# Taking the filler matmuls and the state's identity matmul off TensorE, and adding the state on VectorE instead

## What is computed

```
for t in range(S):                     # B,H,S,D = 4,8,768,48
    new_re = ar * S_re - ai * S_im     # a normalised to |a| <= 0.999, S_* are D x D
    new_im = ar * S_im + ai * S_re
    S_re, S_im = (new_re + outer(k[t], v[t]), new_im)
    y[t] = q[t] @ S_re
x = y as rows (3072 x 384)
x = dense_mixture(x)                   # all 8 experts, normalised gates
out = routed_mixture(x)                # one expert for each row
```

## Time and profile before

| | |
|---|---|
| device time, median of 3 runs | 2652.64 us |
| lowest, highest | 2652.48, 2661.65 us |
| the profiled execution | 2661.65 us, span 2659.8 us |
| mean granted TensorE clock | 0.957 |
| TensorE matmul busy over the span | 2469.9 us (93%) |
| VectorE, ScalarE, GpSimd busy | 1152.1, 748.4, 188.2 us |

### The profile page before, as it was taken

The page is one execution under the profiler, slowest core; times in us unless marked ns, Lnnn a source line. Parts: engine busy times, 40 slices in busy tenths (PEclk is TensorE's granted clock), DMA queues, the critical chain, the costliest instruction groups (busy, mean ns, idle before and its releaser), DMA issues. The chain is left out here.

```text
span 2659.8 us, 41528 instructions
## 1 busy us (share of the span) xinstructions
PE 2469.9 (93%) x14282; PEld 2301.4 (87%) x14283; DVE 1152.1 (43%) x2517; ACT 748.4 (28%) x1293; POOL 188.2 (7%) x176
## 2 busy tenths in 40 slices
PE   0499899999999999999999999999999999599998
PEld 0266666678999999999999999999999999488897
DVE  6876667533444333333333333333333332475433
ACT  4555555332111211211211211211221212254322
POOL 0000000000110110110110110110110100022221
PEclk9988887897999999999999999999999999699999
DMA  3102111110000000000000000000000011243210
GB/s 120 36 29 71 43 66 48 33 34 25 24 25 0 24 25 0 24 24 0 24 24 0 24 24 0 24 24 0 24 24 0 24 37 41 101 144 131 78 38 21
DMA packets 44717, 96.81 MB, mean 36 GB/s; under 512 B 4101, under 2 KB 26651, under 8 KB 44640
## 3 DMA queue, kind: packets, MB, share of 16 engines
q1 hardware_dynamic: 40672, 84.97, 9.4%
q0 software_dynamic: 3968, 10.82, 1.3%
HBM read 161.83 MB, written 10.81 MB: 65 GB/s over the span
## 5 line engine op out<-in xcount | busy, mean ns | idle before, releaser
L986 PE MATMUL bank<-x_parts,w_hi 128*128 (+1 forms) x3072 | 783.4, 335 | 0.1
L871 ACT ACTIVATE h_hi<-bank 128x384 fp32r<-128x384 f32 x512 | 250.2, 492 | 1250.2 <-PE bank L986 1250.1
L986 PEld LDWEIGHTS bank<-x_parts,w_hi 128*128 128x128 f32 x3072 | 554.2, 188 | 0.2 <-DVEq L908 0.2
L940 DVE SCALAR_TENSOR_TENSOR h_lo<-bank,h_hi 128x384 fp32r<-128x384 f32 x512 | 284.1, 557 | 574.5 <-ACT h_hi L871 574.5
L986 PE MATMUL bank<-x_parts,w_lo 128*128 (+1 forms) x1536 | 513.8, 335 | 0.0
L998 PE MATMUL bank<-w_hi,h_hi 128*128 128x384 f32 x1536 | 513.3, 334 | 0.0
L998 PE MATMUL bank<-w_hi,h_lo 128*128 128x384 f32 x1536 | 513.1, 334 | 0.0
L998 PE MATMUL bank<-w_lo,h_hi 128*128 128x384 f32 x1536 | 513.0, 334 | 0.0
L960 DVE SCALAR_TENSOR_TENSOR mixed<-bank,gate,mixed 128x384 f32 (+1 forms) x336 | 207.7, 618 | 444.9 <-PE bank L998 444.9
L986 PEld LDWEIGHTS bank<-x_parts,w_lo 128*128 128x128 f32 x1536 | 289.0, 188 | 0.0
L998 PEld LDWEIGHTS bank<-w_lo,h_hi 128*128 128x128 f32 x1536 | 288.3, 188 | 0.0
(11 more groups left out here) (198 smaller groups left out, 2238.2 us busy)
## 6 DMA issues: line engine op xcount, KB each, us to landing
routed_w_raw<-in_moe_w SPq DMA_DIRECT2D x64, 1536.0 KB, 6.5
w_raw<-in_moe_w SPq DMA_DIRECT2D x32, 768.0 KB, 6.1
q_k<-in_qk SPq DMA_DIRECT2D x24, 512.0 KB, 3.6
decay<-in_a SPq DMA_DIRECT2D x20, 528.0 KB, 5.1
v_rows<-in_v SPq DMA_DIRECT2D x24, 192.0 KB, 2.4
mixed_rows<-mixed SPq DMA_DIRECT2D x4, 1152.0 KB, 4.6
decay<-in_a SPq DMA_DIRECT2D x4, 432.0 KB, 4.8
routed_x<-mixed_rows,gather_now POOLq DMA_INDIRECT x31, 3.1
```

The source lines that it names most:

```text
L871: nc.scalar.activation(h_parts[par][0][:, c, :], h_bank[c], ACT.Relu).then_inc(h_hi, 1)
L940: nc.vector.scalar_tensor_tensor(out=h_parts[par][1][:, c, :], in0=h_bank[c], scalar=0.0, in1=h_parts[par][0][:, c, :].bitcast(F32), op0=A ...
L986: last = nc.tensor.matmul(h_bank[c].rearrange("p (u s) -> p u s", u=SUB), w1_parts[half][w][:, k, c * PT:(c + 1) * PT], mem.x[:, bass.ds(b ...
```

## The change

The identity matmul on the old state goes, and every product of k and v is written to its place in the bank on its own (`start=True, stop=True`). VectorE adds the old state to the bank and writes the sum to a new SBUF tile `state_sum`; the two decay products read that tile (for c = 0 they still read the bank). All filler matmuls go: one for each unit that passes a state on (20) and four for each unit but the last (92).

```diff
+    ssum = mem.at("state_sum", [PT, 2, PAIRS, D], F32, mem.after)
...
-            def await_state_sum(u):
+            def add_state(u):
                 if passes_on(u):
                     dve.wait_ge(kv_done, kept(u) + 1)
+                    if u % NCH:
+                        dve.wait_ge(state_ready, kept(u))
+                        nc.vector.tensor_tensor(ssum[:, :, :, :], state[:, u % 2, :, :, :], kv, ALU.add).then_inc(
+                            state_read, 1)
 
             def decay_state(u, t):
                 if passes_on(u):
                     b, c = divmod(u, NCH)
+                    source = kv
+                    if c:
+                        source = ssum[:, :, :, :]
+                        dve.wait_ge(state_read, kept(u) + 1)
...
-                    nc.vector.tensor_tensor(dst[:, :, :, :], kv, across, ALU.mult).then_inc(state_steps, 1)
-                    if t == IM:
+                    nc.vector.tensor_tensor(dst[:, :, :, :], source, across, ALU.mult).then_inc(state_steps, 1)
+                    if t == IM and not c:
                         dve.wait_ge(state_steps, 2 * kept(u) + 2)
                         dve.sem_inc(state_read, 1)
...
-                await_state_sum(u)
+                add_state(u)
...
-            def keep_warm(bank):
-                nc.tensor.matmul(bank[:, :], ident[:, :], ident[:, :].unsqueeze(1).to_broadcast([PT, BANK // PT, PT]),
-                                 start=True, stop=True)
...
-                                            start=c == 0, stop=c == 0 or (part == IM and h >= H - 2))
+                                            start=True, stop=True)
...
-                    if c:
-                        pe.wait_ge(state_ready, kept(u))
-                        nc.tensor.matmul(kvb[:, 0:2 * PAIRS * D], ident[:, :],
-                                         state[:, u % 2, :, :, :].rearrange("p t g e -> p (t g e)"), start=True, stop=False)
...
-                if passes_on(u):
-                    keep_warm(kt_re)
...
-                if u + 1 < UNITS:
-                    for n in range(4):
-                        keep_warm(sc_a)
```

## The result

The changed kernel takes 2676.65 us (median of 7 executions, 2670.18 to 2681.52) against 2656.33 us before (7 executions, 2652.11 to 2663.74): ratio 1.0072, 95% interval 1.0057 to 1.0086. It is slower by 0.72%, some 19 us. The forecast was 44 us, and a time of 2697.

A forecast was written before the change was run, and what follows sets the result against it. Scan units were taken as bound by the ring through VectorE, ScalarE's squares and odd scores, late units by TensorE. All low +73 us, less 29 for recoveries, gave +44 on 2652.6: about 2697, range 2660 to 2728.

The forecast's parts named there:

- rival A: The forecast itself, chance 0.57: clock low most of the time with short recoveries, 2682 to 2712 us, middle 2697.
- low-clock sums: Unit lengths in units 1 to 23 at the low clock: 15.2 us to the sum of squares plus 11.6 to the mask.
- recovery: Rise of the clock at the sum of squares, 3.2 us at full clock, claimed to save 2.6 us.
- +73: Units 1 to 23 all at the low clock: +39 us in units 1 to 16 and +34 in 17 to 23.
- the ring: Path setting a scan unit's length: odd mask, VectorE, ScalarE's squares, sum of squares, odd scores; addition costs 9 us there.
- one in two: Share of the 22 units with a sum of squares taken to have a recovery, giving back 29 us.
- four in nine: Share of sums of squares begun low or behind a pause that came out at full clock before; worth 25 us.
- Scan and late units: Units 1 to 16, where fillers mostly fill a wait, and 17 to 23, where they stand on the path; all low +39, +34.
- B: Rival, chance 0.15: no recoveries to speak of in the first stage, 68 to 73 us slower, about 2724.
- C: Rival, chance 0.08: clock at full as often as before, its mean above about 0.82; faster, about 2638 us.
- D: Rival, chance 0.14: only scan units fall to low clock, late ones without pauses hold full; +14 us, about 2666.

The follow-up runs named there:

- three_adds: Changed kernel with VectorE's addition of the state done three times in each of 16 units, same output; 2699.62 us, ratio 1.0162 to the kernel before.
- five_adds: Changed kernel with VectorE's addition of the state done five times in each of 16 units, same output; 2714.93 us, ratio 1.0207 to the kernel before.
- split_squares: Changed kernel with the sum of squares split: real part, logits, imaginary part, same work; 2717.42 us, ratio 1.0233 to the kernel before.
- squares_fillers: Kernel before with two more fillers (four in a last chunk) ahead of the sum of squares in units 1 to 17; 2633.08 us, ratio 0.9904.
- hold: Kernel before with squares_fillers' extra fillers plus one ahead of the odd scores in units without an identity matmul; 2620.65 us, ratio 0.9860.

## Why the prediction was wrong in size

**Direction and mechanism.** Slower, by the clock, was right. The mean clock of units 1 to 23 is 0.59 and 0.58, where rival A had near 0.6. Behind the odd scores it is low in 22 of the 23 units from 1 on (all but unit 1; in unit 17 it falls 0.8 us behind the odd mask).

**The low-clock sums.** They are right in the part from the sum of squares to the odd mask: 11.6 us, and the missed units of three_adds and five_adds have 11.64. The part ahead of it was 0.5 us too long, 15.2 where 14.73 was measured; a unit without a recovery comes to 26.4, not 26.8. Unit 11 of the changed kernel, at 0.50, has 25.23 where I had 25.7. Unit 23 has 18.83 us at 0.50 where I had 21.4: that sum seems to have kept the 1.9 us of k transposes, which a last chunk doesn't have. With the lengths as measured (a recovered unit with 2.6 us added), all units low would be +66.7 us and not +73.

**The parts on the ring.** The instruction was sized rightly, 0.55 against 0.54, and the decay products have no change; but I put the 0.55 us on the ring whole (9 us in all), and it costs 0.04. The wait for the release of the bank, which the edit takes away for c > 0, had a part in no sum. The statement that operand sources in SBUF and in the bank take the same 0.55 us had no row of that length behind it; it came out so.

**The step that failed** is the count of recoveries: "I take one in two: 29 us". The changed kernel has 17 in 22, at 2.6 us each, 44 us; and unit 20, between 569.8 and 583.4 us at full clock, took 19.0 us instead of 26.4, 7.4 us more; unit 1, which starts at full clock, is 1.2 us shorter. 66.7 - 44.2 - 7.4 - 1.2 = +13.9, against 13.7 measured in the units of the profiled execution. The size of one recovery was right, 2.6 us; the share of units was off by half as much again, and all of that in the scan units (14 of 16 where I had 8; in the late ones 3 of 6, as taken).

The reason given for one in two was wrong as well: I let the absence of a pause raise the share from four in nine. What decides is how the unit's length stands to the spacing of the clock's rises. In the kernel before, units of 19 to 28 us followed one another, and a share found there says nothing of a kernel whose units are equal: one, two, three, five and seven additions give 9, 8, 4, 5 and 9 hits in nine. That 23.76 us lies just beside the 23.9 between the rises was luck, and nothing in the prediction foresaw it.

**Scan and late units.** I had +19 for the first (39 less 20) and +25 for the others. Measured: -2.3 and +16.0. In the scan units the recoveries (16 us more than taken) and the addition make the difference, in the late ones unit 20 and the sum for unit 23.

**The rivals.** B, no recoveries to speak of, stood at 2724; split_squares, which has hardly any where they count, comes near that state, at 2717. C needed a clock over 0.82. D's time, 2666, is nearer to the result than A's, but its mechanism is the reverse of what happened: it had the loss in the scan units and the late ones at full clock. The late ones lost 16 us at 0.58 while TensorE was busy for 150.92 of 155.41 us. So the row decided against rival D. The Trainium skill's page TensorE: Matmul & The Clock Gate, section Why this matters for your kernels, asks for no idle gaps between bursts of matmuls; this trace shows that here a gap was not needed for the clock to fall and stay low. Where there is a gap the runs agree with it: with the pause filled, in squares_fillers, the clock of units 1 to 16 is 0.95 instead of 0.84, and the kernel 28 us faster.

**Between medians.** The profiled executions show 10 us of the 20. Where the rest lies can't be seen in them and is left open.

## What to carry to other kernels

Before you take filler work off TensorE, or add some, ask at which clock the stretch that ends last will run: a unit of the changed kernel without a recovery comes to 26.4 us, at full clock hold's has 21.9, and the fillers in a wait for another engine cost nothing at full clock, but 2 us of one unit at the low one. A spell of full clock counts only on the stretch that sets the end; two units with clocks of 0.62 and 0.50 had the same 27.8 us. In a loop of equal units don't carry over a share of lucky ones from a kernel with unequal units: follow from unit to unit where the rise falls against the group of matmuls that it should speed up, see whether this distance drifts, and try it by a small delay. And when you add an instruction, look for a wait that goes with the same edit: here it paid for half of the addition, and a short pause of VectorE for most of the rest.

## What the runs showed of the hardware

In units 7 to 10 and 12 to 17 of the changed kernel the clock's rises came 23.9 us apart, each behind the start of the dense 512-column work, and a longer unit can be hit more often than a shorter one: 5 of 9 missed at 24.9 us, none at 27.3. The same instructions in another order cost 1.6% of the kernel (split_squares), with hardly a rise left behind the sum of squares. And amid scores with 64 active rows the clock fell from 2.4 to 1.2 GHz with TensorE busy all the time: four of these scores took 0.71 us at 325.28 and 1.22 us at 328.24. On VectorE, the wait for its own two decay products put 0.70 us between the start of the second and that of the next instruction, 0.47 without it.
